# Windowed attention with routed adapters, one core: part of row 5's adapter product and row 7's first scores moved ahead of row 7's last scores

## What is computed

```python
rel = pos[:, None] - pos[None, :]
mask_plain = (rel >= 0) & (rel < window)
mask_dil = (rel >= 0) & (rel < window * dilation) & (rel % dilation == 0)
scores = np.where(masks[None, :, :, :], scores, -1000000000.0)
attn = np.exp(scores - np.max(scores, axis=-1, keepdims=True))
attn = attn / (np.sum(attn, axis=-1, keepdims=True) + 1e-09)
x = np.matmul(attn, v)
```

```python
logits = x @ w_gate
topk = np.argpartition(-logits, K, axis=1)[:, :K]
w = softmax of the two selected logits
out = x + sum over the two experts e of w[e] * (x @ A[e]) @ B[e]
```

## Time and profile before

| | |
|---|---|
| median of 3 runs | 99.39 us (99.38, 99.39, 100.11) |
| the profiled execution | 100.05 us |
| its span, first to last instruction | 98.3 us |
| busy: TensorE, VectorE, ScalarE, GpSimd | 80.7, 63.4, 71.4, 54.6 us |
| mean granted TensorE clock | 0.977 of full speed |
| data moved | 24.5 MB, mean 249 GB/s |

### The profile page before, as it was taken

One profiled execution on the slowest core, in us unless ns is written; L12 is line 12 of the kernel. 1 busy time (PEld: TensorE's weight loads), 2 busy tenths in 40 slices (PEclk: granted clock), 3 DMA queues, 4 the chain that ended last, 5 costly groups with the idle time before them and its releaser, 6 DMA issues.

```text
span 98.3 us, 3633 instructions
## 1 busy us (share of the span) xinstructions
PE 80.7 (82%) x1587; PEld 59.5 (61%) x1587; DVE 63.4 (65%) x138; ACT 71.4 (73%) x123; POOL 54.6 (56%) x73
## 2 busy tenths in 40 slices
PE   3999968868578989989998989999969989776500
PEld 2443646456455766679776859878757878564300
DVE  5770008606467269448766678789994999979810
ACT  5294791399938992896799598999769989957300
POOL 5999903670459317501945198099184464665820
PEclk9999999999999999999999999999999999999955
DMA  2999999999999999999999999999979999997894
GB/s 38 303 197 198 197 216 209 226 203 216 215 211 214 213 212 216 212 215 216 218 212 214 214 219 211 215 207 205 204 225 416 416 412 420 408 375 287 362 410 194
DMA packets 6095, 24.50 MB, mean 249 GB/s; under 512 B 832, under 2 KB 960, under 8 KB 5440
## 3 DMA queue, kind: packets, MB, share of 16 engines
q0 software_dynamic: 3920, 14.23, 72.7%
q1 hardware_dynamic: 2016, 9.77, 24.4%
q10 hardware_dynamic: 144, 0.28, 0.9%
HBM read 29.07 MB, written 9.44 MB: 392 GB/s over the span
## 4 chain that ended last, share of the span: by engine, by line
PE 30%; DMA 22%; ACT 17%; POOL 11%; DVE 11%; issue 3%; POOLq 0%
PE ps L236 26%; DMA in<-in_qkv_dram 22%; ACT p L374 9%; POOL in L296 7%; DVE x L413 4%; DVE x L574 4%; PE ps L437 3%; POOL xb L420 2%; ACT xt L447 2%; ACT gn L546 2%; POOL x L582 1%; ACT zs L495 1%; ACT gc L543 1%; PE ps L527 1%; DVE rec L410 1%
## 5 line engine op out<-in xcount | busy, mean ns | idle before, releaser
L420 POOL CAST xb<-x 128x1152 bf16<-128x1152 f32 (+1 forms) x16 | 18.3, 1143 | 24.3 <-DVE x L413 24.3
L374 ACT ACTIVATE p<-ps 128x960 bf16<-128x960 f32 (+1 forms) x32 | 27.5, 896 | 3.6 <-PE ps L236 3.3
L236 PE MATMUL ps<-in,p 128*64 128x130 bf16 (+1 forms) x416 | 21.4, 221 | 4.4 <-ACT p L374 3.8
L413 DVE TENSOR_TENSOR x<-ps,rec 128x1152 f32<-128x1152 f32 x16 | 21.7, 1358 | 0.6
L236 PEld LDWEIGHTS ps<-in,p 128*64 128x64 bf16 (+1 forms) x416 | 17.1, 104 | 7.9 <-ACT p L374 5.0
L574 DVE TENSOR_TENSOR x<-x,ps 128x1024 f32<-128x1024 f32 (+1 forms) x16 | 17.5, 1116 | 3.5 <-PE ps L236 3.5
L410 DVE RECIPROCAL rec<-ps 128x18 f32<-128x18 f32 x16 | 4.3, 270 | 16.1 <-PE ps L236 15.9
L522 POOL TENSOR_TENSOR gz<-zs,g 128x640 bf16<-128x640 f32 x7 | 8.9, 1274 | 10.3 <-DVE g L517 10.1
L236 PE MATMUL ps<-warm 128*128 128x512 f32 x22 | 12.2, 693 | 1.5 <-DVE warm L240 1.5
L296 POOL DMA_DIRECT2D in<-in_qkv_dram x22 | 11.8, 581 | 0.8 <-POOLq L710 0.8
L236 PEld LDWEIGHTS ps<-in 64*64 64x64 bf16 x576 | 10.7, 106 | 2.0
(11 more groups left out here) (55 smaller groups left out, 102.7 us busy)
## 6 DMA issues: line engine op xcount, KB each, us to landing
in<-in_qkv_dram POOLq DMA_DIRECT2D x5, 1152.0 KB, 22.8
out_dram<-x SPq DMA_DIRECT2D x5, 1152.0 KB, 8.4
in<-in_qkv_dram POOLq DMA_DIRECT2D x10, 292.5 KB, 23.6
in<-in_qkv_dram POOLq DMA_DIRECT2D x10, 288.0 KB, 8.9
out_dram<-x SPq DMA_DIRECT2D x5, 576.0 KB, 3.0
in<-in_qkv_dram POOLq DMA_DIRECT2D x10, 146.2 KB, 8.2
in<-in_qkv_dram POOLq DMA_DIRECT2D x2, 434.2 KB, 14.5
out_dram<-x SPq DMA_DIRECT2D x1, 320.0 KB, 3.4
```

The source lines that it names most:

```text
L236: return nc.tensor.matmul(o, lhsT=lhsT, rhs=rhs, start=start, stop=stop, skip_group_check=True)
L374: return [nc.scalar.activation(p[:, :, :].rearrange("p h (s c) -> p h s c", c=PER)[:, :, b0 : b0 + nb, 0:SEG], PS[:, k.at : k.at + 2, 0 : ...
L413: nm = add(f"N{tag}", "DVE", ("el", XG), lambda: [nc.vector.tensor_tensor(X[r][:, XG * g : XG * g + XG].rearrange("p (b i n) -> p b i n", ...
L420: add(f"B{tag}", "POOL", ("el", cut), lambda: [nc.gpsimd.tensor_copy(XB[r % 2][:, g, 0:cut], X[r][:, XG * g : XG * g + cut])], [nm] + free)
```

## The change

It moves words in PLAN and one name in REACH. Z05 (with Y05) and S070 (with E070) now stand in front of S171, S071 stands before S170. U5, th4, Cp5 and Cd5 stand in front of T51 and C51. Of row 7's value loads, those of group 0 (Lv700, Lv701) are issued first. The last cut of TensorE's code is in front of S070.

```diff
-    "G2": (8, 7), "V50": (9, 8), "S061": (10, 9), "S171": (None, 10),
+    "G2": (8, 7), "V50": (9, 8), "S061": (10, 9), "S070": (None, 10),
...
-S160@0 A32 Lv710 T50@7 E160 D30@3 S061@5 top4 V60@0 A30 tt4 R60 C50 Lv711
-O1 E061 B51 T51@3 N60 C51 V61@4 th4 g24 R61 N61 U5@7 S171@2 Cp5
-Cd5 S070@0 Z05@7 E171 E070 Z15@6 Y05 S170@2 S071@4 Y15 Lv700 m05 m15 top5
-Lv701 B60 gz4 E170 E071 s125 G4@0 B61 D31@6 tt5 th5 gn4 V70@1 T60@4
+S160@0 A32 Lv700 T50@7 E160 D30@3 S061@5 top4 V60@0 A30 tt4 R60 C50 Lv701
+O1 E061 B51 U5@7 th4 Cp5 Cd5 T51@3 N60 C51 V61@4 g24 R61 N61 Z05@7 Y05
+S070@0 E070 S171@2 E171 Z15@6 Y15 S071@4 S170@2 Lv710 m05 m15 top5
+Lv711 B60 gz4 E170 E071 s125 G4@0 B61 D31@6 tt5 th5 gn4 V70@1 T60@4
```

## The result

The changed kernel takes 99.45 us (median of 22 runs, 99.14 to 100.18), the kernel before in the same series 99.92 us (22 runs, 99.38 to 100.36). The ratio is 0.9961 with a 95% interval of 0.9943 to 0.9979: 0.2 to 0.6 us faster, within 1%. On another occasion, with 12 and 35 runs, the same pair gave 99.60 and 99.70 us, ratio 0.9996 (0.9968 to 1.0025). The gain is therefore small and does not come out in every series.

A forecast was written before the change was run, and what follows sets the result against it. It took Lq711's late landing before S171 as the bound, with blocked g24 as a second delay beside it. Span 98.3 less 0.4 gave 97.9; the median 99.39 less 0.4 gave 99.0 us, range 98.3 to 99.9.

The forecast's parts named there:

- the base of the sum: Whole kernel: 0.4 us is taken from 99.39, the median of the runs, not from the profiled 100.05, giving 99.0.
- Does it reach the end?: From V70 to the last stores: DMA engines have 0.76 us of room, so the whole 0.38 us reaches the end.
- The gap, ScalarE and VectorE: From V61 to V70: Z05 and S070 fill TensorE's 0.77 us gap before S171; V70 starts 0.38 us earlier.
- g24 ahead of B60: After N60: g24 goes first at 70.8 to 70.9 and takes 0.2 us or less instead of 1.08.
- Which part carries the gain: At S171: everything after 72.0 hangs on Lq711's landing; filling the gap there gives at most 0.8 us.
- stores back up: At the end of the kernel: the lower bound of the gain, 0 of the 0.38 us; given no chance.
- Its sign: If stores took V70's 0.4 us gain, the DMA share from 90 to 91 would be near 1.
- The value loads and the cut: Row 7's value-load swap: 0; TensorE's code hop before S070: 0, bounds -0.1 and +3.7 us.
- The second collision: Rival in the tail: top6 goes before GpSimd's A52, some 0.55 us more gained, 98.45 us; chance 0.20.

The follow-up runs named there:

- the kernel with th4 late: The changed kernel with th4 alone put back behind C51 and V61; ratio to the kernel before 1.0047.
- the kernel before with early stores: The kernel before, with stores waiting only for three of row 7's four query-key loads, not for Lq711; ratio to the kernel before 1.0020.
- th4 alone: The kernel before with only th4 moved, in front of T51 and C51; ratio to the kernel before 0.9968.
- resolved on purpose: The changed kernel with S170 in banks 0 and 1 ahead of S071, D31 ahead of G4, and dx5 behind Cp7 and Cd7; ratio to the kernel before 0.9961.
- the kernel with late stores: The changed kernel with stores also waiting for row 7's value loads and O1 moved behind Lv711; ratio to the kernel before 1.0207.
- fourteen profiles: One profiled execution each of the kernel before, the changed kernel, its repeat and the follow-up kernels.

## Why the prediction was right and where it was wrong

Two steps failed: the base of the sum, and "Does it reach the end?".

*The base.* 99.0 was forecast, 99.45 measured, inside the range, and the difference is the base. The three runs shown had a median of 99.39, 22 runs had 99.92, and the later series 99.57 to 99.99. The step that moved the whole sum down to the median of three runs took off 0.66 us from the profiled 100.05; the 22 runs bear out 0.13, the later series up to 0.48. The step from before to after, -0.4% forecast, is -0.39% in the first series and -0.04% in the second. That the first agrees so closely is in part luck: in the profiles the changed kernel's last landing gained 0.01 us and not 0.38.

*The gap, ScalarE and VectorE.* Right, nearly term by term. Forecast from V61's start: Z05 1.18 us later (measured 1.18), S070 1.89 (1.99), S171 2.40 (2.43), Z15 3.08 (3.10), S170 4.38 (4.45), V70 5.88 (5.96). V70's gain from N60, forecast as 0.38 us, was 0.38. It agrees to the hundredth by luck: the way from V61 to V70 was 0.08 us longer than forecast, and V61 started 0.08 us sooner after N60 than before (0.18 instead of 0.26).

*g24 ahead of B60.* Right, and it is the heart of the change. g24 started 0.15 us ahead. In the kernel with th4 late it started 0.05 us behind the cast and took 1.15 us. Both agree with the Trainium skill's rule on the port pair (SBUF — State Buffer, "SBUF: two separate sides"), that the first to start keeps it. That B60 would be held up shows in no row: it starts 0.06 us after N60's end, as before.

*Which part carries the gain.* Wrong. I took the gap for the first cost and th4 for the condition, and wrote that everything after 72.0 hangs on the one landing; the kernel before with early stores has the load 1.3 us sooner and V70 in the same place. It is the release of g24 that must come first: th4 alone gains 0.20 us of V70 by the estimate above when the load lands as in the kernel before, and 0.53 with the load of its own execution. The new order by itself costs 0.24 us of V70, and with th4 it fixes V70 at 6.14 us. Over th4 alone that is a gain only when Lq711 lands later than about 2.2 us after N60.

*Does it reach the end?* Wrong, and this is the step that cost the gain. I read 0.24 busy from 90 to 91 in the earlier trace rows as 0.76 us of room in front of the last stores, and took the whole 0.38 us to the end. The figure is a mean over 16 engines; it can also be 4 engines fully busy and 12 idle. The records do not name the engines, but the number of transfers under way, which hardly reaches zero there and never after the change, speaks for a few that work without a pause; that these hold up the last store is argued, the stream's length from its start is shown. The stores' bound was 25.4 us after their start, 2.48 + 25.4 = 27.9 us after N60, and the compute bound 27.93: the two were equal, and only one was moved. So 0.01 us of the 0.38 reached the end in the first profile and 0.15 in the second. I had named the end "stores back up" as the lower bound, 0, and put no case and no chance on it. Its sign was badly chosen too: the share from 90 to 91 is 1.01 after the change, but only because the execution ran earlier; the low stretch is still there, 0.31 from 88.75 to 89.75.

*The value loads and the cut.* Right: nothing. The packet of the instruction queue came 3.6 us after the hop again. The Trainium skill (Runtime: NRT & Kernel Launch, "Instruction fetch mechanics") lets one expect a stall for a branch out of the two held blocks; neither place of the cut shows one here.

*The second collision.* It did not resolve by itself; top6 stood 0.67 us in the chain as before. When resolved on purpose it moved the last addition by 0.3 us, not 0.55.

## What to carry to other kernels

When a stall goes, look for the second wait at the same join before counting: here a load and a blocked 40-column operation ended within a microsecond of each other, and only the second set the pace in the kernel before, whether the load came early or late. When an edit moves work into another PSUM bank, ask which later group takes that bank next; here it was G4, and it ate the gain. At the end of a kernel keep two sums, the compute chain with the last store's own latency, and the stores from their first issue; a change in one is worth nothing beyond the distance to the other. A mean busy share of many DMA engines is no proof of room.

## What the runs showed of the hardware that was not expected

A store stream of 9.4 MB needed 25.3 to 25.5 us from first issue to last landing in the kernels that it bound, although the mean share fell to 0.31 for a microsecond on the way (88.75 to 89.75 in the changed kernel). In the kernel with late stores the stream ended ragged, with 0.19 and 0.06 of the engines' time in its last two microseconds. Which engines lag, and whether the loads in front give them more to do, was not tried.

Two operations less than 0.2 us apart kept their order in all fourteen profiles: with th4 early g24 started 0.15 us ahead of B60 and took 0.19 us in all eleven, with th4 at its late place it started 0.05 to 0.12 us behind and took 1.08 to 1.15 us in all three.
